# Attention and two MLPs in one kernel: where the weight halves are made, where exponentials and sums are kept, and the order of the second layer

## The reference

```python
# attention: B, H, S, D = 4, 8, 768, 64; chunks of 32 queries, each with 8 memory keys
# and a window of 16 + 32 + 8 keys
scores = scale * np.matmul(q_c, k_full.transpose(0, 1, 3, 2))
scores = scores - np.max(scores, axis=-1, keepdims=True)
a = np.exp(scores)
a = a / (np.sum(a, axis=-1, keepdims=True) + 1e-09)
out[:, :, c_start:c_end] = np.matmul(a, v_full)
# x = its output as 3072 tokens x 512
h = np.maximum(np.maximum(x @ w1, x @ w2), x @ w3)       # w1, w2, w3: 512 x 768
y = h @ w_out                                            # 768 x 512
h = y @ w_in                                             # 512 x 2048
g = np.where(h >= 1, h, np.where(h <= -1, 0.0, (h + 1) ** 2 / 4))
out = g @ w_out2                                         # 2048 x 512
```

## Time and profile before

| | |
|---|---|
| median of 3 runs | 1020.92 us (1016.9 to 1023.32) |
| the profiled execution's own time | 1018.07 us |
| its span, first to last instruction | 1016.3 us |
| mean granted TensorE clock | 0.982 |
| PE busy | 958.1 us (94%) |
| PE weight loads | 886.1 us (87%) |
| DVE busy | 502.8 us (49%) |
| ACT busy | 435.9 us (43%) |
| POOL busy | 458.5 us (45%) |

### The profile page before, as it was taken

The page is one execution under the profiler, slowest core; times in us unless marked ns, Lnnn a source line. Parts: engine busy times, 40 slices in busy tenths (PEclk is TensorE's granted clock), DMA queues, the critical chain, the costliest instruction groups (busy, mean ns, idle before and its releaser), DMA issues.

```text
span 1016.3 us, 19067 instructions
## 1 busy us (share of the span) xinstructions
PE 958.1 (94%) x7806; PEld 886.1 (87%) x7806; DVE 502.8 (49%) x755; ACT 435.9 (43%) x713; POOL 458.5 (45%) x628
## 2 busy tenths in 40 slices
PE   6999999897999999999466999999999999999998
PEld 5999998797989999999466888988889889888897
DVE  4764586878377656740244343354433444332331
ACT  3432343333333334422242454645546555464454
POOL 2669968866176501111889233332432333323321
PEclk9999999999999999999888899999999999999999
DMA  9778999998398927862455544645446344463431
GB/s 359 248 279 277 315 325 381 383 305 347 125 363 295 337 98 270 294 228 86 161 198 187 208 157 166 202 148 209 147 164 236 127 166 140 144 245 117 163 114 62
DMA packets 50327, 223.01 MB, mean 219 GB/s; under 512 B 5952, under 2 KB 10048, under 8 KB 42688
## 3 DMA queue, kind: packets, MB, share of 16 engines
q0 software_dynamic: 31936, 165.17, 46.1%
q1 hardware_dynamic: 18304, 56.63, 15.6%
HBM read 178.00 MB, written 43.78 MB: 218 GB/s over the span
## 4 chain that ended last, share of the span: by engine, by line
PE 81%; POOL 6%; DMA 5%; DVE 4%; issue 3%; ACT 0%; SPq 0%; DVEq 0%; POOLq 0%; ACTq 0%
PE mlp_ps L622 18%; PE mlp_ps L623 17%; PE mlp_ps L624 17%; PE attn_ps L624 3%; PE attn_ps L623 3%; PE attn_ps L622 3%; PE scores_ps L624 3%; PE scores_ps L623 3%; PE scores_ps L622 3%; PE attn_ps L615 2%; DMA wb_scratch<-stage_a 2%; PE trans_ps L624 1%; PE trans_ps L623 1%; PE trans_ps L622 1%; DMA late_raw<-w_in 1%
## 5 line engine op out<-in xcount | busy, mean ns | idle before, releaser
L889 ACT ACTIVATE up_m<-mlp_ps 128x384 f32<-128x384 f32 x293 | 143.5, 490 | 353.9 <-PE mlp_ps L624 322.5
L622 PE MATMUL mlp_ps<-yc,wa 128*128 128x384 f32 x472 | 163.0, 345 | 30.7 <-DMA wb<-wb_scratch 22.4
L623 PE MATMUL mlp_ps<-yc,wa 128*128 128x384 f32 x472 | 160.2, 340 | 0.0
L624 PE MATMUL mlp_ps<-yc,wa 128*128 128x384 f32 x472 | 159.9, 339 | 0.0
L1470 DVE SCALAR_TENSOR_TENSOR ramp<-ramp,up_m 128x768 f32<-128x768 f32 x64 | 63.6, 994 | 136.5 <-ACT ramp L1140 136.5
L503 POOL DMA_DIRECT2D wa<-wa_scratch x59 | 31.8, 539 | 216.4 <-PE mlp_ps L624 212.1
L622 PEld LDWEIGHTS mlp_ps<-yc,wa 128*128 128x128 f32 x472 | 90.0, 191 | 40.9 <-issue 23.3
L622 PE MATMUL mlp_ps<-yc,wb 128*128 128x384 f32 x354 | 119.9, 339 | 1.1 <-DMA wb<-wb_scratch 1.0
L623 PE MATMUL mlp_ps<-yc,wb 128*128 128x384 f32 x354 | 119.2, 337 | 0.0
L624 PE MATMUL mlp_ps<-yc,wb 128*128 128x384 f32 x354 | 118.6, 335 | 0.0
L540 POOL CAST wo<-wo_raw 128x1024 fp32r<-128x1024 f32 x32 | 33.4, 1043 | 178.6 <-PE trans_ps L624 178.6
(11 more groups left out here) (183 smaller groups left out, 2164.8 us busy)
## 6 DMA issues: line engine op xcount, KB each, us to landing
wa<-wa_scratch POOLq DMA_DIRECT2D x59, 1024.0 KB, 5.2
wb<-wb_scratch POOLq DMA_DIRECT2D x59, 768.0 KB, 6.8
qk_raw<-qk_l SPq DMA_DIRECT2D x24, 768.0 KB, 8.2
wo_raw<-w_out POOLq DMA_DIRECT2D x32, 512.0 KB, 4.0
v_raw<-v_l SPq DMA_DIRECT2D x24, 512.0 KB, 6.7
wa_scratch<-stage_a POOLq DMA_DIRECT2D x24, 512.0 KB, 5.5
wb_scratch<-stage_a POOLq DMA_DIRECT2D x24, 384.0 KB, 6.3
y_scratch<-up_m SPq DMA_DIRECT2D x32, 192.0 KB, 1.9
```

The lines of the kernel that those rows point to most:

```text
L622: pe.matmul(out_ap, a_hi, b_hi, start=first, stop=False, skip_group_check=beside)
L623: pe.matmul(out_ap, a_lo, b_hi, start=False, stop=False, skip_group_check=beside)
L624: return pe.matmul(out_ap, a_hi, b_lo, start=False, stop=last, skip_group_check=beside)
L889: return act.activation(o, i, ACT.Copy)
```

## The change

- All 34 halves are made in the first MLP: `HALF_IN` now gives periods 0 to 21 the halves 12 to 33. The single staging slot begins with half 30 in place of 24; halves 28 to 33 have no staging of their own any more.
- The load of wo tile 0 stands in period 23 of layer 1, its split and the load of tile 1 in period 25, and `wo` is two tiles instead of one. The split of tile 1 stands in period 1 of the second MLP and waits until layer 2 is done.
- From the fourth attention group on the exponentials are written to PSUM, over the scores; DVE sums and scales them from there into `prob`. The wait for the transposes goes from ACT to DVE, and the next group's scores wait for the scaled probabilities.
- In the 18 periods that merge into `h_run`, the sums of blocks 0 and 1 are written back into their PSUM bank, and the maximum reads them there. The product that uses such a bank next waits for the maximum (`bank_read`).
- Layer 2 does four of six blocks of outputs 0, 1 and 2, then their last two blocks, then outputs 3 to 7 (`layer2_large`).

```diff
-EARLY, AHEAD, LAST_PAIR, LATE = 4, 12, 24, 28
-HALF_IN = {g: AHEAD + g for g in range(LATE - AHEAD)}
+L2_AHEAD = 3
+EARLY, AHEAD, LAST_PAIR, HALVES = 4, 12, 30, 2 * ITEMS
+HALF_IN = {g: AHEAD + g for g in range(HALVES - AHEAD)}
+WO_LOAD, WO_SPLIT = HALVES - AHEAD + 1, HALVES - AHEAD + 3
...
+        def exp_of(n):
+            if n < GPT:
+                return first_e[n]
+            return scores_of(n)
...
+            def load_wo(g):
+                if g == 0:
+                    for w in w_stored:
+                        pool.wait_ge(w, 32 * ITEMS)
+                else:
+                    pool.wait_ge(wo_split, 2 * g)
+                pool.dma_start(wo_raw[:, :, :].rearrange("p f d -> p (f d)"), w_out2[g % PAIRS]).then_inc(wo_raw_in, 16)
...
+                if g == WO_LOAD:
+                    load_wo(0)
+                if g == WO_SPLIT:
+                    split_wo(0)
+                    load_wo(1)
             for g in range(PERIODS):
-                late = [n for n in (LATE + 2 * g, LATE + 2 * g + 1) if n < 2 * ITEMS]
-                for n in late[0:1]:
-                    split_begin(n)
-                    split_end(n)
-                    load_raw(n + 1)
-                split_wo(g)
...
-                for n in late[1:2]:
-                    split_begin(n)
-                    split_end(n)
...
+                if g:
+                    split_wo(g)
+                    if g + 1 < PERIODS:
+                        load_wo(g + 1)
                 if g + 2 < PERIODS:
                     pool.wait_ge(prod_done, 7 * (g + 1))
                     load_wa(PERIODS_S + g + 2)
...
             def scores_ready(n, j, uses):
                 pe.wait_ge(qk_in[j], 16 * (uses + 1))
-                if not isinstance(n, int) or n >= GPT:
-                    pe.wait_ge(sub_done, n)
+                if n >= GPT:
+                    pe.wait_ge(prob_done, n)
...
+            def bank_read(g, b):
+                if g % 3 and b < 2:
+                    pe.wait_ge(merged, merges(g) + b + 1)
+                else:
+                    pe.wait_ge(summed, 4 * g + b + 1)
...
                 elif q and i < 3:
-                    pe.wait_ge(summed, 4 * (g - 1) + (1, 2, 4)[i])
+                    bank_read(g - 1, (0, 1, 3)[i])
...
+            def layer2_large(v):
+                for x in range(L2_AHEAD):
+                    l2_blocks(v, x, range(KF1 - 2))
+                for x in range(L2_AHEAD):
+                    l2_blocks(v, x, range(KF1 - 2, KF1))
+                for x in range(L2_AHEAD, 2 * KD):
+                    l2_blocks(v, x, range(KF1))
...
-            def exponent(n, slot):
+            def exponent(n):
                 act.wait_ge(sub_done, n + 1)
-                if not isinstance(n, int) or n >= 2:
-                    act.wait_ge(trans_done, n - 1)
-                act.activation(prob[:, slot], score_of(n), ACT.Exp, scale=float(D) ** -0.5).then_inc(exp_done, 1)
+                act.activation(exp_of(n), by_bank(n, score_of(n)), ACT.Exp,
+                               scale=float(D) ** -0.5).then_inc(exp_done, 1)
...
-                to = snap if m else h_run
-                dve.tensor_tensor(to[:, f, t], snap[:, f, t], l1_bank(g, i), ALU.add).then_inc(summed, 1)
+                if m == 0:
+                    to = h_run[:, f, t]
+                else:
+                    to = l1_bank(g, i) if b < 2 else snap[:, f, t]
+                dve.tensor_tensor(to, snap[:, f, t], l1_bank(g, i), ALU.add).then_inc(summed, 1)
...
-                dve.tensor_tensor(h_run[:, f, t], h_run[:, f, t], snap[:, f, t], ALU.max).then_inc(merged, 1)
+                new = l1_bank(g, (3, 5)[b]) if b < 2 else snap[:, f, t]
+                dve.tensor_tensor(h_run[:, f, t], h_run[:, f, t], new, ALU.max).then_inc(merged, 1)
```

More of the change, by code:

```diff
@@ L438, in raw_of @@
             def raw_of(n):
-                return late_raw[:, :] if n >= LATE else w_raw[:, n % 2]
+                return w_raw[:, n % 2]
             def load_raw(n):
@@ L738, in l1_product, with l2_blocks @@
                 last.then_inc(l1_done, 1)
-            def l2_product(v, x):
+            def l2_blocks(v, x, blocks):
                 d, t = l2_part(x)
@@ L745, in l2_product @@
                 reuse = SUBS if v == TILES_S - 1 else 3
[L746 to L749, removed]
-                        pe.wait_ge(summed, 4 * (last_pair + 1))
[L751 to L759, removed]
+                if blocks[0] == 0:
+                    if x >= reuse:
+                        pe.wait_ge(y_copied, y_before(v) + x - reuse + 1)
+                    elif v == TILES_S - 1:
+                        if x == SUBS - 1:
+                            pe.wait_ge(summed, 4 * (last_pair + 1))
+                    elif x < 2:
+                        bank_read(last_pair, x)
+                    else:
+                        pe.wait_ge(summed, 4 * (last_pair + 1))
+                for f in blocks:
+                    if x == 0 and f == 0:
+                        pe.wait_ge(h2_lo_done, 4 * f0)
+                    if x < 2 and f >= KF1 - 2:
+                        pe.wait_ge(h2_lo_done, 4 * f0 + 2 * (f - KF1 + 2) + x + 1)
                     wc = slice(f * DM + d * P, f * DM + (d + 1) * P)
@@ L762, in l2_product @@
                                  f == 0, f == KF1 - 1)
-                last.then_inc(l2_done, 1)
+                if blocks[-1] == KF1 - 1:
+                    last.then_inc(l2_done, 1)
+            def layer2_large(v):
[5 more added lines that the diff above has]
+                    l2_blocks(v, x, range(KF1))
             def strassen_tile(v):
@@ L806, in _ @@
                 if v + 1 < TILES_S:
-                    for x in range(2 * KD):
-                        l2_product(v, x)
+                    layer2_large(v)
             def product(g, i):
@@ L862, in _ @@
             product(0, 1)
-            for x in range(2 * KD):
-                l2_product(TILES_S - 1, x)
+            layer2_large(TILES_S - 1)
             for i in range(2, 7):
@@ L1216, in softmax_shift, with softmax_scale @@
                                   ALU.subtract).then_inc(sub_done, 1)
-            def softmax_scale(n, slot, e):
+            def softmax_scale(n, slot):
+                e = exp_of(n)
+                pair, rec = row_pair[:, :, 0], row_rec[:, :]
+                if n < GPT:
+                    rec = rec.unsqueeze(2).to_broadcast([P, H, WIN])
+                else:
+                    pair = pair.rearrange("p (r j) -> p r j", r=2)
+                    rec = rec.rearrange("p (r j) -> p r j", r=2).unsqueeze(3).to_broadcast([P, 2, HALF_HEADS, WIN])
                 dve.wait_ge(exp_done, n + 1)
-                dve.tensor_reduce(row_pair[:, :, 0], e, X, ALU.add).then_inc(sum_done, 1)
+                dve.tensor_reduce(pair, e, X, ALU.add).then_inc(sum_done, 1)
                 dve.wait_ge(sum_done, n + 1)
@@ L1270, in first_tile @@
                         slot = (n0 + j) % 2
-                        softmax_scale(n0 + j, slot, prob[:, slot])
+                        softmax_scale(n0 + j, slot)
                     if f < len(weights):
```

86 lines of the change are left out of this document (33 added, 53 removed).

## The result

The changed kernel takes 975.13 us in the median of 4 runs (971.97 to 977.86), the kernel before 1018.91 us beside it. The ratio is 0.958 (95% interval 0.951 to 0.965). The forecast was 973 us, in a range of 961 to 988. The span of the profiled run is 972.1 us, 44.2 less than before.

The account below looks back on a forecast made before the run. TensorE was taken as the bound, with time to win only where it idles or runs at half clock. Gains 36.6 + 11 + 3.5 less 3.5 lost made 47.6 us, so 973 us from the 1020.92 median; range 961 to 988.

Parts of the forecast that it names:

- Part 1: Second MLP, periods 1 to 4: without the late halves they take 62.2 us in place of 98.84, gaining 36.6 us.
- its lower bound: Second MLP, periods 1 to 4: gain of only 32 us if half clock returns after the short period.
- Part 2: Tiles 1 and 2 of the first MLP: six more halves there cost 3.5 us, bounds 0 and 10.
- a slot that makes loads late: Tile 2: single-slot rounds of 10 us against 7.35 us periods; the fourth load is 2.8 us over its slack.
- excess transfers: Tile 2: 3.0 MB a period, 410 GB/s against 368 in tile 0, an excess of 3.4 us over four periods.
- Part 3: First MLP: PSUM maxima save 8.0 us of VectorE work in tile 0, scaling exponentials from PSUM saves 2.1 us.
- 11 + 3.5 us: Tiles 0 and 1: gains taken of 14.1 us lost in tile 0 and 4.25 us in tile 1.
- The free write into PSUM: Merging periods of the first MLP: writing sums back into their PSUM bank was taken to cost nothing extra.
- the price of the maximum: First MLP: a maximum with one input in PSUM takes 550 ns, against 1219 ns from SBUF in tile 0.
- Part 4: Layer 2: reordering removes VectorE waits of 3.12 us and 1.7 us of half clock in tile 0.
- Transfers did not take VectorE's place in tile 0: Rival: transfers limit tile 0, which gains only layer 2's 4.8 us; 979.5 us in all, chance 0.15.
- Its low end, 961: Whole kernel: all of tiles 0 and 1 comes back, tile 2 loses nothing, and the wo wait goes.

Follow-up runs that it names:

- e1: Changed kernel with the maxima, exponentials and layer 2 order undone, halves and first wo split kept, waits on h's low halves one by one; 994.72 us, ratio 0.977.
- e3: Changed kernel with the exponentials written to prob in SBUF and scaled there, as before the change; 980.70 us, ratio 0.964.
- e7: Changed kernel with POOL's arithmetic for halves 30 to 33 on one column, same loads and stores, output wrong; 973.10 us, ratio 0.956.
- e10: Changed kernel with two staging slots and POOL's arithmetic on one column for halves 30 to 33, full transfers, output wrong; 972.60 us, ratio 0.956.
- e4: Changed kernel with layer 2 in the old order, each output's six blocks together, finer waits on h_lo kept; 978.14 us, ratio 0.962.
- e2: Changed kernel with all sums going to SBUF again and all maxima reading two SBUF tiles; 983.05 us, ratio 0.966.
- e5: Changed kernel with two staging slots by turns for halves 30 to 33, same transfers and POOL work; 976.19 us, ratio 0.960.
- e8: Changed kernel with loads and stores of halves 30 to 33 cut to 4 columns, POOL's arithmetic whole, output wrong; 974.99 us, ratio 0.958.

## Why the prediction was right, and where it was not

- **Part 1 (36.6 us).** Right in mechanism and size: 35.8 us, and e1 shows that the halves alone give it. The 98.84 us it started from is 0.46 too long, as its cut at 578.83 is POOL's load and not period 5's first matmul. A period lasts 15.64 us again from period 2 on. The half clock that its lower bound allowed for shows in e3's profile only, where it costs 1.5 us.
- **Part 2 (3.5 us lost, bounds 0 and 10).** The loss is 6.6 us. The step that failed is what PE would wait for. I worked out a slot that makes loads late, and excess transfers. The first is real (its three rounds last 10.8, 10.3 and 11.3 us from one load of wa to the next, against the 10 taken), but in the changed kernel PE waits only 1.5 us for loads, in the tile's sixth period, and 3.7 when POOL's arithmetic is taken away (e7); of the transfers' rate 0.4 us show at most (e10). The cause that I left out is my own part 3's: POOL's arithmetic in tile 2 holds off the two-input instructions that stay on VectorE, which had 554 ns there only because POOL was idle. I moved the work and did not ask whom it would hold off in its new place.
- **Part 3 with tiles 0 and 1 (11 + 3.5 us, with part 4).** The sum was right, 12.3 + 3.4 us. The free write into PSUM was right (560 ns), and so was the price of the maximum (554 against the 550 taken). Its split was not: undone singly, the maxima are worth 9.0 us over both tiles, the exponentials 5.3 (I had taken 2.1 of VectorE time in tile 0, which was about right, 2.8, but not that PE waits on it, which the trace of the kernel before showed: 2.3 us), the order 3.2. These were worth more in the changed kernel than against the kernel before, since the halves alone made tile 1 8.6 us longer (e1). The forecast took tile 1's 111.62 us as what the new schedule starts from; it was not. That tile 1's 3.5 us came out is luck: the halves cost 8.6 us there, and the other parts took 12.0 off again. The halves, with the finer waits that e1 keeps, give 22 us (1016.95 less 994.72) of some 42, the rest of the change 20.
- **Part 4.** The wait on h_lo is gone from both layer 2s and the half clock with it, as predicted. From its first matmul layer 2 takes 25.84 us in tile 0 (30.84 before) and 24.96 in tile 1 (26.62 before), 5.0 us less in tile 0 against the 4.8 counted. The new order alone is not all of it: with the old order and the finer waits e4 loses 1.2 us of these 5.0, and e1, with slow maxima ahead, 2.5. With the new order layer 2 takes 25.84 and 24.96 us in e2 too, with its slow maxima.
- **Rivals.** Transfers did not take VectorE's place in tile 0: PE waits 0.6 us on wb there, at a DMA share of 1.02. They are close to it, though. In e5 and e8, whose tile 0 is the changed kernel's, PE waited 2.5 us for wa, and tile 0 took 110.46 and 112.32 us. The line of e8:

```profile
PE mlp_ps L623 <- DMA wa<-wa_scratch: 2.5, 1, 2.5
```

- **Range.** Its low end, 961, comes out only from the profiled run's 1018.07; from the median of 1020.92, which the forecast starts from, the same terms give 964.

## What to carry to other kernels

Work on GpSimd that reads SBUF is not free when the bound is elsewhere: ask which VectorE instructions with two SBUF inputs it meets at its new place, and what waits behind them. Move such work to a stage in which VectorE's queue has slack (layer 2 here), or give VectorE's critical instructions one input in PSUM. When one delay hides another, taking away either moves little; only both together tell.

## What the runs showed of the hardware

A 128 x 384 sum written into PSUM takes 560 ns, against 550 into SBUF (tile 2 of the changed kernel). The maximum of the earlier trace rows, with two SBUF inputs, took 2.95 us for 0.55 us of work beside POOL's low halves; with one input in PSUM each of tile 0's twelve took 553 to 557 ns. This agrees with what the Trainium skill states (SBUF — State Buffer, "Who interferes with whom"): a VectorE instruction with two SBUF inputs contends with a GpSimd instruction that reads SBUF, one with at most one SBUF input does not. In the trace one wait outlasted two such GpSimd instructions, and it hit a maximum that had begun at 194.84, 0.25 us before the first of them:

```profile
195.09 1.30 POOL L484 TENSOR_TENSOR stage_a<-w_raw,stage_a 128x512 fp32r<-128x512 f32 x1
196.34 1.02 POOL L486 TENSOR_TENSOR stage_a<-stage_a 128x384 fp32r<-128x384 f32 x1
```

A wait for one slow store can move such a meeting away from where it hurts: periods 12 to 15 of tile 1 took 37.2 us with the single slot and 40.7 with two (e1). That the slot alone makes this difference was not tried.
